# The first layer of a mixture of experts with weights standing and 128 tokens moving

## The chip, the cores and the metric

The program runs on one core of a Trainium2 chip. The metric is the device time in microseconds (us) of the whole program. Of its engines, TensorE (PE) multiplies, VectorE (DVE) and ScalarE (ACT) do arithmetic along partitions, GpSimd (POOL) starts gathers and scatters, and SyncE (SP) starts the plain transfers. In the profile PEld is the part of TensorE that loads the operand that stands.

## The reference: what is computed

Attention over 2 x 8 heads gives 1536 tokens of 512 numbers. A first mixture of 8 experts (two per token) follows, and then a second one, which is what the change touches. Its core is:

```python
def _moe2_ref(x, w_skip, w_gate, w1, w2):       # x 1536 x 512, w1 8 x 512 x 1024, w2 8 x 1024 x 512
    do_compute = x @ w_skip > 0                 # tokens that are computed at all
    out = x.copy(); xc = x[do_compute]
    logits = xc @ w_gate
    e_idx = np.argmax(logits, axis=1)           # one expert per token
    probs = softmax(logits); gate_w = probs[np.arange(len(xc)), e_idx]
    for e in range(8):
        mask = e_idx == e
        h = np.maximum(xc[mask] @ w1[e], 0.0)   # first layer: 1024 units
        y[mask] = gate_w[mask, None] * (h @ w2[e])
    out[do_compute] = xc + y
```

## The kernel before

Each engine has its own instruction list, written by hand in program order, and the lists meet at semaphores. No scheduler reorders anything. After the attention (to about 90 us of the profiled span), the routing of the first mixture (to 114 us), the first mixture (to 437 us) and the second routing (to 477 us), the second mixture runs to the end.

All products of the two mixtures are made from operands in the type F32R. A number is split in two: ACT rounds it to F32R (hi), DVE takes the rest (lo), and three products hi x hi, hi x lo and lo x hi are summed. Numbers of plain f32 are used only for turns (a product with the identity, which transposes 128 x 128) and for the small products of the routing.

The second mixture works in slots. A slot is up to 128 tokens of one expert; an expert with more tokens has more slots, and a register loop runs over them. In one slot, for the 128 tokens, PE does this (`second_mixture`, lines 951 to 1008):

1. First layer, `up`: for each of FH = 2 halves of 512 units, 12 products (4 chunks of the 512 inputs x 3 terms). The tokens stand (128 inputs x 128 tokens, `xt_hi`, `xt_lo`) and 512 columns of weights move. The result has tokens on partitions and 512 units along them, in one PSUM bank (`ps_h[half]`).
2. `turn_h`: the second layer sums over units, so these must lie on partitions. ACT applies the ReLU into `h_sb` (line 1282), PE turns four 128 x 128 pieces into `ps_ht[half]` (line 980), ACT rounds this into `ht_hi[half]` (line 1285) and DVE takes the rest into `ht_lo[half]` (line 1963). The turns of half 0 stand in the middle of the products of half 1, those of half 1 in the middle of the second layer's.
3. Second layer, `down`: 24 products, where `ht_hi` and `ht_lo` stand and 512 columns of the second weights move, into `ps_y`. Within it stands `turn_x` (line 936): the next slot's gathered rows `xg` are turned into `ps_xt`, which ACT rounds into `xt_hi` (line 1254) and of which DVE takes the rest into `xt_lo` (line 1935).

The helpers `terms` and `products` list the operands and issue the products; all of them have line 964. Before the first products of a slot PE waits only for half of `xt_hi`, after six for the other half, and for `xt_lo` before the last four of half 0. DVE then scales `ps_y` into `y_sb` (line 1973), and POOL scatters it. Beside this, ACT and DVE prepare the next expert's weights in 8 pieces (`round_next`, line 1097, and `split_next`, line 1615), placed between the steps of the slot by the table SLOT_PIECES = (2, 1, 2, 3).

Of the kernel before, what the change touches and what calls it, by code (L numbers as in the profile page):

```python
# [31 lines left out]
ALU = mybir.AluOpType  # L32
ACT = mybir.ActivationFunctionType
AX = mybir.AxisListType

P = 128
BATCH, HEADS, SEQ, HD = 2, 8, 768, 64
D = HEADS * HD
# [15 lines left out]
DK = D // P  # L54
FK = FF // P
FH = FF // D
# [95 lines left out]
def build(nc, q, k, v, gates1, gates2, noise, m1_w1, m1_w2, m2_w1, m2_w2, const, out):  # L152
# [14 lines left out]
    with keep:  # L167
# [3 lines left out]
        def sb_in(stack, name, shape, dt=F32):  # L171
            return stack.enter_context(nc.sbuf_tensor(name, shape, dt))
# [5 lines left out]
        bank = [keep.enter_context(nc.psum_tensor(f"bank{i}", [P, 512], F32))[:] for i in range(4)]  # L178
# [8 lines left out]

        TAIL = 2
        ps_gate_tail = bank[0]
        ps_h, ps_ht, ps_y, ps_xt = bank[0:2], bank[2:4], bank[4], bank[5]  # L190

        ps_unit, ps_out, ps_x, ps_turn = bank[0:2], bank[2:5] + [bank[6]], bank[5], bank[7]

# [10 lines left out]
        def c(name):  # L204
# [7 lines left out]
        ident = c("ident")  # L212
# [63 lines left out]
        routing = ExitStack()  # L276
# [32 lines left out]
        second = ExitStack()  # L309
        xt_b = [sb_in(second, f"xt_b{i}", [P, DK, P]) for i in range(2)]  # L310
        second.close()
        h_sb = sb_in(routing, "h_sb", [P, FH, D])
        ht_hi, ht_lo = [sb_in(routing, f"ht_{part}", [P, FH, DK, P], F32R) for part in ("hi", "lo")]
        xt_hi, xt_lo = [sb_in(routing, f"xt_{part}", [P, DK, P], F32R) for part in ("hi", "lo")]
        xg = sb_in(routing, "xg", [P, ROW])
# [92 lines left out]
            "gate": "DVE: the slot's gates are in gate_next (one more than slots)",  # L408
            "gated": "DVE: they are in gate_now",
            "h": "PE: one more half of the hidden layer",  # L410
            "relu": "ACT: in h_sb",
            "ht": "PE: transposed",
            "hth": "ACT: rounded, in ht_hi",
            "hte": "DVE: the rest is in ht_lo",
            "y": "PE: the expert's output (one more than slots)",
            "ix": "DVE: the slot's destinations are in ix_put",
            "set": "ACT: one more set of weights is free",
# [241 lines left out]
        def _(eng):  # L659
# [261 lines left out]
            def second_mixture():  # L921
                m, S = 1, slot_sems
                eng.sem_inc(S["xtp"], 1)
                eng.sem_inc(S["y"], 1)
                slot = eng.alloc_register(f"pe_slot{m}")
                eng.reg_mov(slot, 0)
                counts = [eng.alloc_register(f"pe_blocks{m}_{e}") for e in range(E)]
                done = eng.alloc_register(f"pe_done{m}")

                def turn_x(ahead, n):  # L930

                    eng.wait_ge(S["take"], (n + (ahead + 1)) * 16)
                    if ahead:
                        eng.wait_ge(S["xte"], n + ahead)
                    for i in range(DK):
                        last = eng.transpose(ps_xt[:, i * P:(i + 1) * P], xg[:, i * P:(i + 1) * P],  # L936
                                             ident)
                    last.then_inc(S["xtp"], 1)

                eng.wait_ge(s_counted, m + 1)  # L940
                eng.reg_load(counts, todo_i[0:1, 0:E])
                keep_warm(10, ps_y)
                turn_x(0, 0)

                eng.wait_ge(s_route, m + 1)
                for e in range(E):
                    n = m * E + e
                    hi, lo = w_hi[n % SETS], w_lo[n % SETS]
                    eng.wait_ge(s_lo, PIECES * n - PIECES // 2)
                    eng.reg_mov(done, 0)  # L950
                    with eng.While(lambda: eng.snap(done) < eng.snap(counts[e])):
                        sv = eng.snap(slot, min_val=0, max_val=2 * NT + E)

                        def terms(x_hi, x_lo, chunks):


                            with_hi = [(x_hi[i], w[:, chunk, :]) for i, chunk in enumerate(chunks)
                                       for w in (hi, lo)]
                            return with_hi + [(x_lo[i], hi[:, chunk, :])
                                              for i, chunk in enumerate(chunks)]  # L960

                        def products(ps, every, a, b):
                            for i in range(a, b):
                                last = eng.matmul(ps[:], *every[i], start=(i == 0),  # L964
                                                  stop=(i == len(every) - 1))
                            return last

                        xs = [[x[:, i, :] for i in range(DK)] for x in (xt_hi, xt_lo)]
                        up = [terms(*xs, [FH * i + half for i in range(DK)]) for half in range(FH)]
                        down = []  # L970
                        for half in range(FH):
                            hs = [[h[:, half, i, :] for i in range(DK)] for h in (ht_hi, ht_lo)]
                            down += terms(*hs, [WC // 2 + half * DK + i for i in range(DK)])
                        T = 3 * DK
                        H = 2 * DK

                        def turn_h(half):
                            eng.wait_ge(S["relu"], sv * 2 + (half + 1))
                            for i in range(DK):
                                last = eng.transpose(ps_ht[half][:, i * P:(i + 1) * P],  # L980
                                                     h_sb[:, half, i * P:(i + 1) * P], ident)
                            last.then_inc(S["ht"], 1)

                        eng.wait_ge(S["xth"], sv * 2 + 1)
                        products(ps_h[0], up[0], 0, H // 2)
                        eng.wait_ge(S["xth"], sv * 2 + 2)
                        products(ps_h[0], up[0], H // 2, H)
                        eng.wait_ge(S["xte"], sv + 1)
                        products(ps_h[0], up[0], H, T).then_inc(S["h"], 1)
                        products(ps_h[1], up[1], 0, T // 2)  # L990
                        turn_h(0)
                        products(ps_h[1], up[1], T // 2, T).then_inc(S["h"], 1)
                        eng.wait_ge(S["hth"], sv * 2 + 1)
                        eng.wait_ge(s_lo, PIECES * n)
                        eng.wait_ge(S["ye"], sv + 1)
                        products(ps_y, down, 0, T // 2)
                        turn_h(1)
                        products(ps_y, down, T // 2, H)
                        eng.wait_ge(S["hte"], sv * 2 + 1)
                        products(ps_y, down, H, T)  # L1000
                        eng.wait_ge(S["hth"], sv * 2 + 2)
                        products(ps_y, down, T, T + T // 3)
                        turn_x(1, sv)
                        products(ps_y, down, T + T // 3, T + H)
                        eng.wait_ge(S["hte"], sv * 2 + 2)
                        products(ps_y, down, T + H, 2 * T).then_inc(S["y"], 1)
                        eng.reg_add(slot, slot, 1)
                        eng.reg_add(done, done, 1)
# [68 lines left out]
        def _(eng):  # L1077
# [166 lines left out]
            def second_mixture():  # L1244
                m, S = 1, slot_sems
# [23 lines left out]
                for e in range(E):  # L1269
# [7 lines left out]
                    with eng.While(lambda: eng.snap(done) < eng.snap(counts[e])):  # L1277
                        sv = eng.snap(slot, min_val=0, max_val=2 * NT + E)
                        round_next(n, 0)
                        for half in range(FH):  # L1280
                            eng.wait_ge(S["h"], sv * 2 + (half + 1))
                            eng.activation(h_sb[:, half, :], ps_h[half][:], ACT.Relu)\
                               .then_inc(S["relu"], 1)
                            eng.wait_ge(S["ht"], sv * 2 + (half + 1))
                            eng.copy(ht_hi[:, half].rearrange("p k n -> p (k n)"), ps_ht[half][:])\
                               .then_inc(S["hth"], 1)
                            round_next(n, half + 1)
                        round_x(1, sv)
                        round_next(n, 3)
                        eng.reg_add(slot, slot, 1)  # L1290
                        eng.reg_add(done, done, 1)
# [278 lines left out]
        def _(eng):  # L1570
# [351 lines left out]
            def second_mixture():  # L1922
                m, S = 1, slot_sems
                eng.sem_inc(S["ye"], 1)
                slot = eng.alloc_register(f"dve_slot{m}")
                eng.reg_mov(slot, 0)
                counts = [eng.alloc_register(f"dve_blocks{m}_{e}") for e in range(E)]
# [22 lines left out]
                for e in range(E):  # L1950
# [3 lines left out]
                    with eng.While(lambda: eng.snap(done) < eng.snap(counts[e])):  # L1954
# [5 lines left out]
                        split_next(n, 0)  # L1960
                        for half in range(FH):
                            eng.wait_ge(S["hth"], sv * 2 + (half + 1))
                            eng.tensor_tensor(
                                ht_lo[:, half].rearrange("p k n -> p (k n)"), ps_ht[half][:],
                                ht_hi[:, half].bitcast(F32).rearrange("p k n -> p (k n)"),
                                ALU.subtract).then_inc(S["hte"], 1)
                            split_next(n, half + 1)
                        rest_of_x(1, sv)
                        split_next(n, 3)
# [84 lines left out]
```

## Time and profile before

| | us |
|---|---|
| time, median of 3 runs (lowest, highest) | 666.77 (666.35, 667.37) |
| time of the profiled execution | 665.87 |
| its span, from the first to the last instruction | 663.4 |
| PE busy in it | 620.8 (94%) |
| PEld busy | 551.5 (83%) |
| DVE busy | 367.9 (55%) |
| ACT busy | 293.9 (44%) |
| POOL busy | 237.9 (36%) |
| mean granted TensorE clock | 0.97 of full |

The span is cut in no stages by the profile; a stage is found by the lines that are active in it. A row of the timeline has its start, its length, the engine, the line, the operation, and the operands as out<-in; for a product the first operand after the arrow moves and the second stands, and "128x512" is the shape that moves. Products overlap in the pipe, so what one costs is the distance between the starts of two neighbours and not the length shown.

### The profile page before, as it was taken

To read this page: it belongs to the slowest core of one execution; us is meant where nothing else is said; L and a number is where in the kernel's file an instruction comes from. 1 tells how busy PE (TensorE), PEld (TensorE's weight loads), DVE (VectorE), ACT (ScalarE), POOL (GpSimd) and SP (SyncE) were. 2 spreads that over 40 slices of the span, in tenths; PEclk is the share of its full clock that TensorE was granted. 3 is DMA by queue.
4 is the path that set the end of the run, shared out by engine and by line. 5 is a ranking of instruction groups with operands and counts; after the bars stand their busy time and mean duration, and the time that the engine had idled before them with its cause. 6 is when DMAs were issued, how large, how long until landed. Compare 5 with 4: busy or idle time off the path is not lost.

```text
span 663.4 us, 13555 instructions
## 1 busy us (share of the span) xinstructions
PE 620.8 (94%) x4054; PEld 551.5 (83%) x4054; DVE 367.9 (55%) x714; ACT 293.9 (44%) x536; POOL 237.9 (36%) x223
## 2 busy tenths in 40 slices
PE   6888848999999999999999999998699999999994
PEld 6567735999999999999999999985478888888883
DVE  5759985644535554364644536423564687656641
ACT  2657732433424443253433434433255475646621
POOL 2558303105527063370725527033112223231230
PEclk9999967999999999999999999998699999999998
DMA  9999881442926448283672926885296679568220
GB/s 305 326 285 305 301 295 53 155 152 55 269 66 180 140 93 264 54 213 94 150 207 54 273 65 157 236 251 113 72 330 208 208 220 357 160 187 266 40 50 13
DMA packets 57633, 119.79 MB, mean 181 GB/s; under 512 B 13588, under 2 KB 13972, under 8 KB 57568
## 3 DMA queue, kind: packets, MB, share of 16 engines
q1 hardware_dynamic: 39424, 94.59, 43.4%
q0 software_dynamic: 14304, 23.93, 17.2%
q10 hardware_dynamic: 3840, 0.49, 0.5%
q8 instruction: 30, 0.49, 0.3%
q14 instruction: 35, 0.29, 0.1%
HBM read 103.51 MB, written 23.50 MB: 191 GB/s over the span
## 4 chain that ended last, share of the span: by engine, by line
PE 84%; DMA 5%; DVE 4%; issue 2%; SPq 2%; POOLq 0%; ACT 0%; POOL 0%; DVEq 0%; ACTq 0%
PE bank L964 22%; PE bank L856 22%; PE bank L850 22%; PE bank L839 2%; DMA q_ring<-in_q 2%; PE bank L819 2%; PE bank L745 2%; PE bank L980 2%; PE bank L724 1%; DMA xg<-x_moe,ix_take 1%; PE bank L768 1%; PE bank L758 1%; PE bank L713 1%; PE bank L936 1%; DVE col_val L1778 1%
## 5 line engine op out<-in xcount | busy, mean ns | idle before, releaser
L1615 DVE TENSOR_TENSOR w_lo<-stage,w_hi x120 | 141.7, 1222 | 22.9 <-ACT w_hi L1097 22.1
L1097 ACT CAST w_hi<-stage x120 | 119.7, 1050 | 9.0 <-PE bank L964 8.9
L856 PE MATMUL bank<-unit_hi,w_hi 128*128 128x416 f32 x256 | 92.6, 362 | 0.0
L1873 DVE SCALAR_TENSOR_TENSOR unit_lo<-bank,unit_hi 128x416 fp32r<-128x416 f32 x64 | 37.9, 592 | 96.8 <-ACT unit_hi L1211 96.8
L850 PE MATMUL bank<-tok_hi,w_hi 128*128 128x416 f32 x256 | 90.5, 354 | 0.6 <-DVE tok_lo L1825 0.6
L1211 ACT ACTIVATE unit_hi<-bank 128x416 fp32r<-128x416 f32 x64 | 33.2, 519 | 129.9 <-PE bank L850 129.9
L856 PE MATMUL bank<-unit_lo,w_hi 128*128 128x416 f32 x256 | 90.2, 352 | 0.0
L850 PE MATMUL bank<-tok_hi,w_lo 128*128 128x416 f32 x256 | 89.7, 350 | 0.0
L856 PE MATMUL bank<-unit_hi,w_lo 128*128 128x416 f32 x256 | 89.7, 350 | 0.0
L1429 POOL DMA_INDIRECT x_more<-more_out,ix_put x32 | 51.6, 1614 | 42.2 <-DVE more_out L1844 26.3
L1441 POOL DMA_INDIRECT x_moe<-rows_out,ix_put x32 | 55.2, 1726 | 9.8 <-issue 9.8
L850 PE MATMUL bank<-tok_lo,w_hi 128*128 128x416 f32 x256 | 58.5, 350 | 0.0
L1409 POOL COPY ix_take<-take_ix 128x4 int32 (+1 forms) x8 | 1.5, 184 | 135.2 <-PE bank L819 135.2
L850 PEld LDWEIGHTS bank<-tok_hi,w_hi 128*128 128x128 f32 x256 | 48.0, 188 | 1.5 <-issue 1.0
L856 PEld LDWEIGHTS bank<-unit_hi,w_hi 128*128 128x128 f32 x256 | 48.1, 188 | 1.0
L856 PEld LDWEIGHTS bank<-unit_hi,w_lo 128*128 128x128 f32 x256 | 48.3, 189 | 0.5
L850 PEld LDWEIGHTS bank<-tok_hi,w_lo 128*128 128x128 f32 x256 | 48.1, 188 | 0.4
L856 PEld LDWEIGHTS bank<-unit_lo,w_hi 128*128 128x128 f32 x256 | 48.0, 188 | 0.4
L850 PEld LDWEIGHTS bank<-tok_lo,w_hi 128*128 128x128 f32 x256 | 47.9, 187 | 0.5
L964 PE MATMUL bank<-w_hi,ht_hi 128*128 128x512 f32 x112 | 46.7, 417 | 0.0
L964 PE MATMUL bank<-w_hi,xt_hi 128*128 128x512 f32 x112 | 45.6, 407 | 0.5 <-ACT xt_hi L1254 0.5
L964 PE MATMUL bank<-w_lo,ht_hi 128*128 128x512 f32 x112 | 44.3, 395 | 0.0
(162 smaller groups left out, 1072.5 us busy)
## 6 DMA issues: line engine op xcount, KB each, us to landing
stage<-in_moe_w SPq DMA_DIRECT2D x128, 512.0 KB, 5.6
v_win<-in_v SPq DMA_DIRECT2D x24, 198.0 KB, 8.9
v_raw<-in_v SPq DMA_DIRECT2D x6, 528.0 KB, 13.4
x_moe<-rows_out SPq DMA_DIRECT2D x12, 260.0 KB, 3.6
kt<-in_k SPq DMA_DIRECT2D x8, 384.0 KB, 9.0
q_ring<-in_q SPq DMA_DIRECT2D x6, 512.0 KB, 9.6
x_att<-x_sb POOLq DMA_DIRECT2D x12, 256.0 KB, 5.8
x_part<-x_moe SPq DMA_DIRECT2D x4, 768.0 KB, 8.8
```

The source lines that it names most:

```text
L745: last = eng.matmul(ps_heads[part, h, 0:HD + 1], pt_sb[:, s % 2, i, part], v_win[:, (2 * t + half) % WR, h * VD:(h + 1) * VD], start=True, ...
L819: last = eng.transpose(ps[:, i * rows:(i + 1) * rows], rows_in[0:rows, t, i * P:(i + 1) * P], ident[0:rows, 0:rows])
L839: last = eng.transpose(ps_turn[0:PART[t], t * P:(t + 1) * P], out_t[:, PSTART[t]:PSTART[t] + PART[t]], ident)
L850: last = eng.matmul(ps_unit[f % 2][:, 0:W], w, x, start=(i == 0), stop=(i == len(mine) - 1))
L856: last = eng.matmul(ps_out[chunk][:, 0:W], w[:, WC // 2 + f, chunk * P:(chunk + 1) * P], h[:, f % UNITS, :], start=(f == 0 and i == 0), st ...
L964: last = eng.matmul(ps[:], *every[i], start=(i == 0), stop=(i == len(every) - 1))
L1097: eng.copy(piece(w_hi[n % SETS], j), stage[:, j, :]).then_inc(s_hi, 1)
L1211: eng.activation(unit_hi[:, f % UNITS, :], ps_unit[f % 2][:, 0:W], ACT.Relu)\
L1429: eng.indirect_dma_start(more_dram, bass.IndirectOffsetOnAxis(ap=ix_put[0:rows, t:t + 1], axis=0), more_out[0:rows, t, :], None, bounds_ch ...
L1441: eng.indirect_dma_start(x1_dram, bass.IndirectOffsetOnAxis(ap=ix_put[0:rows, t:t + 1], axis=0), rows_out[0:rows, t, :], None, bounds_chec ...
L1615: eng.tensor_tensor(piece(w_lo[n % SETS], j), stage[:, j, :], piece(w_hi[n % SETS], j).bitcast(F32), ALU.subtract)\
L1873: eng.scalar_tensor_tensor(unit_lo[:, f % UNITS, :], ps_unit[f % 2][:, 0:W], 0.0, unit_hi[:, f % UNITS, :].bitcast(F32), ALU.max, ALU.subt ...
```

## The change

In the first layer the operands trade places. For each half and each of its four groups of 128 units, 12 products are made in which a 128 x 128 piece of the weights stands and the 128 tokens move, into 128 columns of `ps_h[half]`. The result has units on partitions, so that `turn_h`, `h_sb`, `ps_ht` and the semaphores "relu" and "ht" go. ACT applies the ReLU and rounds to F32R in one instruction from `ps_h`, and DVE takes max(x, 0) - hi from the same bank. PE now waits for all of `xt_hi` and `xt_lo` before its first product, and for DVE to have read `ps_h[half]` of the slot before; ACT waits for the last slot's output before it writes `ht_hi`.

```diff
@@ PE, second_mixture
-                        xs = [[x[:, i, :] for i in range(DK)] for x in (xt_hi, xt_lo)]
-                        up = [terms(*xs, [FH * i + half for i in range(DK)]) for half in range(FH)]
+                        def units(half):
+                            for at in range(0, D, P):
+                                every = [(w[:, FH * i + half, at:at + P], x[:, i, :])
+                                         for x, ws in ((xt_hi, (hi, lo)), (xt_lo, (hi,)))
+                                         for i in range(DK) for w in ws]
+                                for i, (w, x) in enumerate(every):
+                                    last = eng.matmul(ps_h[half][:, at:at + P], w, x, start=(i == 0),
+                                                      stop=(i == len(every) - 1))
+                            last.then_inc(S["h"], 1)
...
-                        eng.wait_ge(S["xth"], sv * 2 + 1)
-                        products(ps_h[0], up[0], 0, H // 2)
                         eng.wait_ge(S["xth"], sv * 2 + 2)
-                        products(ps_h[0], up[0], H // 2, H)
                         eng.wait_ge(S["xte"], sv + 1)
-                        products(ps_h[0], up[0], H, T).then_inc(S["h"], 1)
-                        products(ps_h[1], up[1], 0, T // 2)
-                        turn_h(0)
-                        products(ps_h[1], up[1], T // 2, T).then_inc(S["h"], 1)
+                        eng.wait_ge(S["hte"], sv * 2 + 1)
+                        units(0)
+                        eng.wait_ge(S["hte"], sv * 2 + 2)
+                        units(1)
                         eng.wait_ge(S["hth"], sv * 2 + 1)
                         eng.wait_ge(s_lo, PIECES * n)
                         eng.wait_ge(S["ye"], sv + 1)
-                        products(ps_y, down, 0, T // 2)
-                        turn_h(1)
-                        products(ps_y, down, T // 2, H)
-                        eng.wait_ge(S["hte"], sv * 2 + 1)
+                        products(ps_y, down, 0, H)
+                        eng.wait_ge(S["hte"], sv * 2 + 3)
                         products(ps_y, down, H, T)
@@ ACT, second_mixture
                             eng.wait_ge(S["h"], sv * 2 + (half + 1))
-                            eng.activation(h_sb[:, half, :], ps_h[half][:], ACT.Relu)\
-                               .then_inc(S["relu"], 1)
-                            eng.wait_ge(S["ht"], sv * 2 + (half + 1))
-                            eng.copy(ht_hi[:, half].rearrange("p k n -> p (k n)"), ps_ht[half][:])\
-                               .then_inc(S["hth"], 1)
+                            eng.wait_ge(S["y"], sv + 1)
+                            eng.activation(ht_hi[:, half].rearrange("p k n -> p (k n)"), ps_h[half][:],
+                                           ACT.Relu).then_inc(S["hth"], 1)
@@ DVE, second_mixture
-                            eng.tensor_tensor(
-                                ht_lo[:, half].rearrange("p k n -> p (k n)"), ps_ht[half][:],
+                            eng.scalar_tensor_tensor(
+                                ht_lo[:, half].rearrange("p k n -> p (k n)"), ps_h[half][:], 0.0,
                                 ht_hi[:, half].bitcast(F32).rearrange("p k n -> p (k n)"),
-                                ALU.subtract).then_inc(S["hte"], 1)
+                                ALU.max, ALU.subtract).then_inc(S["hte"], 1)
```

On PE, in the second half of the first layer and the start of the second, this stood in a row before (w_hi and w_lo are the weights' two parts, xt the tokens, ht the turned hidden layer, h_sb the layer not yet turned):

```order
L964 MATMUL bank<-w_hi,xt_hi 128x512
L964 MATMUL bank<-w_lo,xt_hi 128x512
L964 MATMUL bank<-w_hi,xt_hi 128x512
L964 MATMUL bank<-w_lo,xt_hi 128x512
L964 MATMUL bank<-w_hi,xt_hi 128x512
L964 MATMUL bank<-w_lo,xt_hi 128x512
L980 MATMUL bank<-c_late,h_sb 128x128 x4
L964 MATMUL bank<-w_hi,xt_hi 128x512
L964 MATMUL bank<-w_lo,xt_hi 128x512
L964 MATMUL bank<-w_hi,xt_lo 128x512 x4
L964 MATMUL bank<-w_hi,ht_hi 128x512
```

And this stands on PE now for the last 128 units of the second half and the start of the second layer:

```order
L966 MATMUL bank<-xt_hi,w_hi 128x128
L966 MATMUL bank<-xt_hi,w_lo 128x128
L966 MATMUL bank<-xt_hi,w_hi 128x128
L966 MATMUL bank<-xt_hi,w_lo 128x128
L966 MATMUL bank<-xt_hi,w_hi 128x128
L966 MATMUL bank<-xt_hi,w_lo 128x128
L966 MATMUL bank<-xt_hi,w_hi 128x128
L966 MATMUL bank<-xt_hi,w_lo 128x128
L966 MATMUL bank<-xt_lo,w_hi 128x128 x4
L972 MATMUL bank<-w_hi,ht_hi 128x512
L972 MATMUL bank<-w_lo,ht_hi 128x512
```

Twelve products of 512 moving columns for 512 units became four such groups of twelve, with 128 moving columns each, and the operand that stands changes from tokens to weights; the turns are gone.

On ACT, from a slot's first to its last step of its own, this stood before (the pieces of the next weights, which stand between, are left out of this last expert's slot):

```order
L1282 ACTIVATE h_sb<-bank 128x512
L1285 CAST ht_hi<-bank 128x512
L1281 REGISTER_ALU
L1282 ACTIVATE h_sb<-bank 128x512
L1285 CAST ht_hi<-bank 128x512
L1252 REGISTER_ALU
L1254 CAST xt_hi<-bank 128x256 x2
```

and this now:

```order
L1276 REGISTER_ALU
L1277 ACTIVATE ht_hi<-bank 128x512
L1275 REGISTER_ALU
L1277 ACTIVATE ht_hi<-bank 128x512
L1246 REGISTER_ALU
L1248 CAST xt_hi<-bank 128x256 x2
```

Two of ACT's four passes over the hidden layer are gone, and the one left in each half writes `ht_hi` itself.

## Rows read from the trace of the kernel before

**Rows 1.** The page: the chain that ended last, shares of the span by line.

```profile
PE bank L964 22%; PE bank L856 22%; PE bank L850 22%; PE bank L839 2%; DMA q_ring<-in_q 2%; PE bank L819 2%; PE bank L745 2%; PE bank L980 2%; PE bank L724 1%; DMA xg<-x_moe,ix_take 1%; PE bank L768 1%; PE bank L758 1%; PE bank L713 1%; PE bank L936 1%; DVE col_val L1778 1%
```

**Rows 2.** Busy by stretch: length, PE, PEld, DVE, ACT, POOL, clock, DMA, GB/s.

```profile
489.80:652.80 163.00, 163.00 (x782) 132.44 (x781) 100.30 (x143) 87.44 (x129) 44.20 (x39) 1.00 0.61 192
33.00:83.00 50.00, 43.80 (x707) 36.96 (x705) 41.56 (x71) 33.72 (x93) 29.97 (x41) 1.00 0.95 298
472.60:474.50 1.90, 1.84 (x4) 1.49 (x5) 0.66 (x3) 0.00 (x0) 1.10 (x1) 0.50 0.00 0
```

**Rows 3.** Chain of waits, one slot: start us, us, what.

```profile
502.33 6.07 PE bank L964 x26
508.84 2.81 PE bank L964 x12
514.85 6.08 PE bank L964 x26
```

**Rows 4.** Groups by form on PE: count, busy us, mean ns.

```profile
L964 PE MATMUL bank<-w_hi,xt_hi 128*128 128x512 f32 x112 | 45.6, 407 | 0.5 <-ACT xt_hi L1254 0.5
L980 PE MATMUL bank<-c_late,h_sb 128*128 128x128 f32 x112 | 16.8, 273 | 0.0
```

**Rows 5.** Timeline, slot 2: start us, us, engine, line, operation.

```profile
491.54 0.39 PE L964 MATMUL bank<-w_hi,xt_hi 128*128 128x512 f32 x1
...
493.17 0.39 PE L964 MATMUL bank<-w_lo,xt_hi 128*128 128x512 f32 x1
...
496.06 0.19 PEld L964 LDWEIGHTS bank<-w_hi,xt_hi 128*128 128x128 f32 x1
496.17 0.19 PEld L964 LDWEIGHTS bank<-w_lo,xt_hi 128*128 128x128 f32 x1
496.41 0.40 PE L964 MATMUL bank<-w_lo,xt_hi 128*128 128x512 f32 x1
```

**Rows 6.** Timeline of the first mixture, 416 columns a product.

```profile
124.16 0.19 PEld L856 LDWEIGHTS bank<-unit_hi,w_lo 128*128 128x128 f32 x1
124.35 0.35 PE L856 MATMUL bank<-unit_hi,w_lo 128*128 128x416 f32 x1
```

**Rows 7.** Timeline: plain f32 products, 16 columns moving.

```profile
38.10 0.97 PEld L758 LDWEIGHTS bank<-wgate,xt_a 128*128 128x128 f32 x8
```

**Rows 8.** Timeline: plain f32 products, 128 columns moving.

```profile
441.29 1.04 PE L768 MATMUL bank<-xt_b,wgate 128*9 128x128 f32 x8 [0.24 <-ACT xt_b L1174]
```

**Rows 9.** Weight loads by line: ns min/median/max, first and last start.

```profile
L693 PEld LDWEIGHTS bank<-w_hi x30: 186/330/338, 104.8 to 476.2; 128*128 128x128 f32 x30
...
L758 PEld LDWEIGHTS bank<-wgate,xt_a x96: 186/192/338, 33.2 to 88.1; 128*128 128x128 f32 x96
```

**Rows 10.** Timeline: tokens of slot 3, from their turn to their use.

```profile
502.37 0.65 ACT L1254 CAST xt_hi<-bank 128x256 fp32r<-128x256 f32 x2 [2.17 <-PE bank L936]
503.13 0.68 DVE L1935 TENSOR_TENSOR xt_lo<-bank,xt_hi 128x512 fp32r<-128x512 f32 x1
504.05 0.40 PE L964 MATMUL bank<-w_hi,xt_hi 128*128 128x512 f32 x1
```

**Rows 11.** Timeline: the first slot's start, and the wait within it.

```profile
478.11 0.50 PE L964 MATMUL bank<-w_hi,xt_hi 128*128 128x512 f32 x1 [0.46 <-ACT xt_hi L1254]
478.45 0.68 DVE L1935 TENSOR_TENSOR xt_lo<-bank,xt_hi 128x512 fp32r<-128x512 f32 x1
...
489.16 0.66 PE L936 MATMUL bank<-c_late,xg 128*128 128x128 f32 x4 [0.56 <-DMA xg<-x_moe,ix_take]
```

**Rows 12.** ACT and DVE by form, within one slot.

```profile
L1963 DVE TENSOR_TENSOR ht_lo<-bank,ht_hi 128x512 fp32r<-128x512 f32 x2 | 1.4, 692 | 1.5 <-ACT ht_hi L1285 1.5
...
L1282 ACT ACTIVATE h_sb<-bank 128x512 f32<-128x512 f32 x2 | 1.2, 604 | 0.3 <-PE bank L964 0.3
L1285 ACT CAST ht_hi<-bank 128x512 fp32r<-128x512 f32 x2 | 1.2, 588 | 2.4 <-PE bank L980 2.4
```

**Rows 13.** The page: the same DVE form, from the first mixture.

```profile
L1873 DVE SCALAR_TENSOR_TENSOR unit_lo<-bank,unit_hi 128x416 fp32r<-128x416 f32 x64 | 37.9, 592 | 96.8 <-ACT unit_hi L1211 96.8
```

More of the change, by code:

```diff
@@ L189, in build @@
         ps_gate_tail = bank[0]
-        ps_h, ps_ht, ps_y, ps_xt = bank[0:2], bank[2:4], bank[4], bank[5]
+        ps_h, ps_y, ps_xt = bank[0:2], bank[4], bank[5]
         ps_unit, ps_out, ps_x, ps_turn = bank[0:2], bank[2:5] + [bank[6]], bank[5], bank[7]
@@ L311, in build @@
         second.close()
-        h_sb = sb_in(routing, "h_sb", [P, FH, D])
         ht_hi, ht_lo = [sb_in(routing, f"ht_{part}", [P, FH, DK, P], F32R) for part in ("hi", "lo")]
@@ L410, in build @@
             "h": "PE: one more half of the hidden layer",
-            "relu": "ACT: in h_sb",
-            "ht": "PE: transposed",
             "hth": "ACT: rounded, in ht_hi",
-            "hte": "DVE: the rest is in ht_lo",
+            "hte": "DVE: the rest is in ht_lo (two more)",
             "y": "PE: the expert's output (one more than slots)",
@@ L952, in second_mixture, with terms @@
                         sv = eng.snap(slot, min_val=0, max_val=2 * NT + E)
-                        def terms(x_hi, x_lo, chunks):
-                            with_hi = [(x_hi[i], w[:, chunk, :]) for i, chunk in enumerate(chunks)
+                        def terms(h_hi, h_lo, chunks):
+                            with_hi = [(h_hi[i], w[:, chunk, :]) for i, chunk in enumerate(chunks)
                                        for w in (hi, lo)]
-                            return with_hi + [(x_lo[i], hi[:, chunk, :])
+                            return with_hi + [(h_lo[i], hi[:, chunk, :])
                                               for i, chunk in enumerate(chunks)]
+                        def units(half):
[7 more added lines that the diff above has]
+                            last.then_inc(S["h"], 1)
                         def products(ps, every, a, b):
@@ L975, in second_mixture @@
                         H = 2 * DK
[L977 to L982, printed above, removed]
-                        eng.wait_ge(S["xth"], sv * 2 + 1)
-                        products(ps_h[0], up[0], 0, H // 2)
                         eng.wait_ge(S["xth"], sv * 2 + 2)
-                        products(ps_h[0], up[0], H // 2, H)
                         eng.wait_ge(S["xte"], sv + 1)
-                        products(ps_h[0], up[0], H, T).then_inc(S["h"], 1)
-                        products(ps_h[1], up[1], 0, T // 2)
-                        turn_h(0)
-                        products(ps_h[1], up[1], T // 2, T).then_inc(S["h"], 1)
+                        eng.wait_ge(S["hte"], sv * 2 + 1)
+                        units(0)
+                        eng.wait_ge(S["hte"], sv * 2 + 2)
+                        units(1)
                         eng.wait_ge(S["hth"], sv * 2 + 1)
@@ L1004, in second_mixture @@
                         products(ps_y, down, T + T // 3, T + H)
-                        eng.wait_ge(S["hte"], sv * 2 + 2)
+                        eng.wait_ge(S["hte"], sv * 2 + 4)
                         products(ps_y, down, T + H, 2 * T).then_inc(S["y"], 1)
@@ L1924, in second_mixture @@
                 eng.sem_inc(S["ye"], 1)
+                eng.sem_inc(S["hte"], 2)
                 slot = eng.alloc_register(f"dve_slot{m}")
```

## The prediction, made before the result was known

> **What bounds the kernel now.** I read the shares of the chain of waits first. It names PE lines at its head, and the line of the second mixture's products (964) has 22% of the span [rows 1]. Then the busy time by stretch: in the 163.00 us that hold 13 slots PE is busy 163.00, at a granted clock of 1.00 (the higher of its two levels, 2.4 GHz), while DVE has 100 and ACT 87 [rows 2]. So a slot is as long as PE's own instructions, and any time put on PE or taken off it in a slot moves the end by the same. The chain of one slot shows this: from 502.33 to 514.85 it is PE with no gap of another engine worth a row, 12.52 us [rows 3]. The number of slots: the product of w_hi with xt_hi occurs 8 times a slot (2 halves x 4 chunks) and 112 times in all [rows 4], so there are 14 slots.
>
> **What a 512-column product and a turn cost.** The lengths shown overlap, so I take distances. From 491.54 to 493.17 there are seven steps: 1.63 / 7 = 0.233 us [rows 5]. A slot has 48 such products, 11.18 us. The other 12.52 - 11.18 = 1.34 us are 12 turns, 0.112 us each.
>
> **What goes from PE.** 24 products of the first layer, 24 x 0.233 = 5.59 us, and the eight turns of `turn_h` (8 x 14 = 112, as counted [rows 4]), 8 x 0.112 = 0.90 us. Together 6.49 us a slot.
>
> **What comes to PE.** 2 halves x 4 groups x 12 = 96 products with 128 columns moving and 128 x 128 F32R standing. The arithmetic is the same as that of the 24; if only columns counted, a product would cost 0.233 / 4 = 0.058 us. But each one needs another piece to stand, so 96 loads stand where 24 stood, and before, the 512 columns that moved hid each load. The trace has no F32R product with fewer than 416 columns, so its price must be bounded.
> - From below: 0.058 us, by columns alone.
> - By the load: after the turns, where PE has two loads to make at once, two F32R loads start at 496.06 and 496.17, so one load holds the next up for 0.11 us [rows 5]. Plain f32 pieces of the same 128 x 128, with only 16 columns moving, show it better: eight loads take 0.97 us [rows 7], the last one alone 0.19 (median 192 ns [rows 9]), so their starts are (0.97 - 0.19) / 7 = 0.111 us apart.
> - From above: plain f32 with 128 columns moving has two records a product, and eight records take 1.04 us [rows 8], so a product costs 0.22 (starts apart, with the last one's 0.27 us taken off, the length of a 128-column product [rows 4]) to 0.26 us.
>
> I take 0.111, the nearest row: same piece standing, same bytes, few columns moving. 96 x 0.111 = 10.66 us.
>
> On this the Trainium skill's page "TensorE: Matmul & The Clock Gate" (section "Back-to-back issue gap") speaks more kindly: in a sustained stream of loads and products it gives about 81 ns for each product of 128 columns. By it the 96 would cost 7.8 us, an estimate, and not 10.66. The trace has only spacings of 0.11 for 128 columns of 4-byte numbers, so I keep it as a rival.
>
> **The sum.** A slot gains 10.66 - 6.49 = 4.17 us on PE, 14 slots 58.4 us.
>
> **Edits off PE.** ACT loses two passes a slot (588 ns each) and keeps two (604); DVE's pass keeps its cost: the subtraction takes 692 ns for 512 columns [rows 12], the form that is new here took 592 for 416 in the first mixture [rows 13]. ACT and DVE have room, 87 and 100 us of 163 [rows 2], and a longer slot gives more. This is hidden work: 0.
>
> **New waits.** PE's first product now waits for all of `xt_lo`, and everything of PE is queued behind it. In slot 3 the rounding starts 502.37, the rest 503.13 and lasts 0.68, to 503.81; the first product of the slot starts 504.05 [rows 10]. The stretch behind `turn_x` on PE (8 products) stays, so the 0.24 us of slack stays. In slots where DVE's pieces of weights delayed the rest, they stood behind a half that itself waited for a turn; that turn is gone, so they come sooner. I take 0, and at most 0.3 us a slot, 4 us in all. Below nothing it cannot go, since a wait gives nothing back. In the first slot the start moves: product at 478.11, `xt_lo` ready at 478.45 + 0.68 = 479.13 [rows 11], so 1.0 us more. Its wait of 0.56 us for gathered rows at 489.16 [rows 11] goes, because PE now comes there some 4 us later. Net 0.5. The wait for `ps_h` is for a read that ended in the slot before; ACT's new wait for "y" is met when the products that it reads begin. Both 0.
>
> Total 58.4 + 0.5 = 58.9 us. The profiled execution took 665.87 us, so 724.8; the median of the runs is 0.9 higher, so about **725.7 us**.
>
> **Rivals.**
> - *Columns price it, not slower.* If loads hid fully, 0.058 x 96 = 5.6 us against 6.49, so 0.9 less a slot, 12.9 us in all: 654 us. It takes the place of the load's cost in the first layer, and decides below 6.49 / 96 = 0.0676 us a product. For it: nowhere in the mixture did a load cost anything. Against: both spacings of 0.11. Chance 0.03.
> - *Loads partly hidden.* A product costs between 0.0676 and 0.10 us, because F32R loads pipeline better than the plain ones; with 0.081 it is 7.78 - 6.49 = 1.29 a slot, 18 us: 685 us. Against it stands the 0.11 of the two F32R loads themselves. Chance 0.06. It would take the page's figure to be right for 4-byte pieces.
> - *Loads in series.* In the first mixture a load starts at 124.16, lasts 0.19, and its product starts at 124.35 [rows 6]; if a load may not start before the product before it, and must end before its own, the spacing is 0.19. Then 96 x 0.19 = 18.2, 11.7 more a slot, 164 in all: 831 us. Against it: 496.06 and 496.17, two loads that overlap, and the eight of [rows 7]. Chance 0.08.
> - *F32R is fast only with many columns moving.* All 128-column products of 4-byte numbers here cost like plain ones, and all F32R products shown move 416 or 512. If 128 columns fall back to the price of plain f32, 0.22 us a product, a slot gains 21.1 - 6.49 = 14.6 us, 205 in all: 872 us. For it: nothing here excludes it. Against: no row shows such a fall. Chance 0.24. The Trainium skill's page "FP8 and Floating Point Precision" (section "TensorE Precision Notes") gives plain f32 four passes and has reduced f32 read 4 bytes and cut them to 22 bits, with no word on columns; by it the 872 would not come, and the sum would stay with the load. No run so far shows which.
> - *The clock falls.* The moving side is now at work about half the time of the first layer (0.058 of 0.111). With the clock at 0.50 [rows 2] an F32R load has 330 ns instead of 186 [rows 9]; twice the spacing, 0.222 us, again gives 872 us. Against: in the attention, with short products all along and PE busy 43.8 of 50 us, the clock was 1.00 [rows 2]. Chance 0.03.
>
> **How the numbers follow.** The forecast has 0.56. Its own range: 0.108 to 0.120 us a product (0.120 being the F32R surplus that 0.233 has over 512 columns at 2.4 GHz, 9%, laid on the load) and 0 to 4 us of waits, so 720 to 742 us. The two slow prices hold 0.35 with the clock's, so a range that leaves out 2 in 10 must reach them: 716 to 885 us, 0.91 of the chance, the lower rivals left out. Faster by over 0.2% (about what a measurement of this kernel can tell from no change) only in the first rival, part of it: 0.02. Within 0.2%: 0.01. Slower: 0.97, which all others share.
>
> **What would show it.** Right: in the first layer starts 0.11 us apart, load behind load, PE busy all through, slots of 16.7 us, the granted clock at 1.00, the second layer's products still 0.233 apart, no waits on ACT or DVE at a slot's start but for the first. Wrong: a first layer of about 5.6 us (columns), 18 (series) or 21 (plain price); lengths of records that grow from 0.27 us tell the plain price from the load, since a longer pass shows in the product and a longer load in PEld. The step on which all hangs is the 0.111.

## The result, and the profile after

The changed kernel takes 735.51 us (median of 4 runs, 734.39 to 738.41), the kernel before 667.07 us on the same chip (4 runs, 666.35 to 668.41). The ratio is 1.106, with a 95% interval of 1.103 to 1.110. The forecast was 726 us with a range of 716 to 885. All ratios in this document are of executions within 1.5% of the fastest one of their kernel.

The page of the changed kernel: the shares of the chain by line, and the groups of the new first layer on PE, PEld, DVE and ACT (out<-in, count, busy us, mean ns, idle before).

```profile
PE bank L966 22%; PE bank L853 20%; PE bank L847 20%; PE bank L972 11%; PE bank L836 2%; PE bank L742 2%; PE bank L816 2%; PE bank L721 2%; PE bank L710 1%; DMA v_raw<-in_v 1%; PE bank L755 1%; PE bank L765 1%; PE bank L672 1%; PE bank L933 1%; DVE col_val L1770 1%
...
L966 PE MATMUL bank<-xt_hi,w_hi 128*128 128x128 f32 x448 | 110.3, 283 | 1.6 <-DVE xt_lo L1928 1.6
L966 PEld LDWEIGHTS bank<-xt_hi,w_hi 128*128 128x128 f32 x448 | 89.9, 201 | 4.1 <-issue 4.1
...
L1956 DVE SCALAR_TENSOR_TENSOR ht_lo<-bank,ht_hi 128x512 fp32r<-128x512 f32 x28 | 19.4, 691 | 89.3 <-ACT ht_hi L1277 89.3
...
L1277 ACT ACTIVATE ht_hi<-bank 128x512 fp32r<-128x512 f32 x28 | 16.8, 598 | 118.0 <-PE bank L966 118.0
```

The products of the first layer (now line 966, 22% of the span) and of the second (972, 11%) stand in the chain in place of the common line 964, which had 22% [rows 1]. DVE's new form takes 691 ns against 692 before, and ACT's one pass 598 ns [rows 12]. Both engines wait more than before, and behind the first slot's start they hold up PE nowhere (the 1.6 us that PE waits for `xt_lo` in line 966 are all at that start): the edits off PE cost nothing, as forecast.

The chain of waits from the first slot into the third (start us, us, what):

```profile
477.07 0.69 DVE xt_lo L1928
477.88 19.87 PE bank L966 x96
497.75 6.10 PE bank L972 x16
506.17 10.67 PE bank L966 x96
516.84 3.78 PE bank L972 x16
521.06 1.86 PE bank L972 x8
522.92 10.68 PE bank L966 x96
```

From 506.17 to 522.92 one slot takes 16.75 us: 10.67 for 96 products (0.111 each), 5.64 for 24 of 512 columns (3.78 and 1.86), the rest the four turns of the tokens. It took 12.52 us before [rows 3]. All the later slots look alike, 16.77 us on average. The first slot does not: from 477.88 to 506.17 it takes 28.29 us.

PEld in a later slot, four loads of the first layer in a row (start us, us):

```profile
539.43 0.19 PEld L966 LDWEIGHTS bank<-xt_hi,w_hi 128*128 128x128 f32 x1 [0.16 <-issue]
539.55 0.19 PEld L966 LDWEIGHTS bank<-xt_hi,w_lo 128*128 128x128 f32 x1
539.66 0.19 PEld L966 LDWEIGHTS bank<-xt_hi,w_hi 128*128 128x128 f32 x1
539.77 0.19 PEld L966 LDWEIGHTS bank<-xt_hi,w_lo 128*128 128x128 f32 x1
```

The starts are 0.11 us apart while each load is shown with 0.19: loads overlap, and a new one starts every 0.11 us. That the product waits for its load, and not for something else that costs 0.11 us, is what the table by columns below is for. Before, the same two starts, 0.11 apart, stood only where PE came out of its turns [rows 5].

The granted clock on PE in the first slot (window, length, PE busy and count, PEclk, DMA share, GB/s):

```profile
core 0: us, PE busy (x), PEclk, DMA share, GB/s
475.00:476.00 1.00, 1.00 (x6) 0.78 0.01 4
477.00:478.00 1.00, 0.12 (x1) 1.00 0.83 262
478.00:479.00 1.00, 1.00 (x10) 0.93 1.06 393
479.00:480.00 1.00, 1.00 (x6) 0.50 1.08 342
480.00:484.00 4.00, 4.00 (x21) 0.50 1.00 301
504.00:508.00 4.00, 4.00 (x30) 1.00 0.33 115
```

The clock rises to 1.00 (2.4 GHz) between 475 and 476, in the last of the ten wide products that warm PE up ahead of the slots. PE idles for 1.6 us, until 477.88. Its clock is still 1.00 then, falls to 0.50 (1.2 GHz) at about 479, and stays there through all of the narrow products; it is back by 504, after products of 512 columns have run from 497.6. The 96 products take 19.87 us there and not 10.67, and the second layer's first 16 take 6.10 and not 3.78. In all later slots the clock is at 1.00 (columns: length, PE, PEld, DVE, ACT, POOL, PEclk, DMA share, GB/s):

```profile
506.17:722.00 215.83, 215.83 (x1604) 200.41 (x1603) 100.05 (x140) 70.79 (x100) 42.15 (x38) 1.00 0.45 133
```

So the 69.5 us between the two profiled executions (735.36 - 665.87) are: 13 later slots, 13 x (16.77 - 12.54) = 55.0, where 12.54 is the 163.00 us of [rows 2] over 13; the first slot, 28.13 against 13.43, 14.7; an earlier start, 477.88 against 478.11, -0.2. Both lengths of the first slot are from its first product to that of the second slot: to 506.01 now, where the chain's piece begins 0.16 later, and from 478.11 to 491.54 before, with the wait for gathered rows in it [rows 5, 11].

### The profile page after: what moved, and what is told of

It is laid out like the page before. It is cut to its first block, busy times and chain, and to the rows that moved or that the text cites. A ratio compares the mean times of both kernels' runs of the same rounds, so it can differ in the third digit from the quotient of the medians.

```text
span 732.9 us, 15376 instructions
## 1 busy us (share of the span) xinstructions
PE 690.1 (94%) x4950; PEld 637.4 (87%) x4950; DVE 371.6 (51%) x714; ACT 278.1 (38%) x508; POOL 236.2 (32%) x223
## 4 chain that ended last, share of the span: by engine, by line
PE 89%; DVE 4%; DMA 3%; issue 2%; SPq 1%; ACT 0%; POOLq 0%; POOL 0%; DVEq 0%; ACTq 0%
PE bank L966 22%; PE bank L853 20%; PE bank L847 20%; PE bank L972 11%; PE bank L836 2%; PE bank L742 2%; PE bank L816 2%; PE bank L721 2%; PE bank L710 1%; DMA v_raw<-in_v 1%; PE bank L755 1%; PE bank L765 1%; PE bank L672 1%; PE bank L933 1%; DVE col_val L1770 1%
## 5 line engine op out<-in xcount | busy, mean ns | idle before, releaser
L966 PE MATMUL bank<-xt_hi,w_hi 128*128 128x128 f32 x448 | 110.3, 283 | 1.6 <-DVE xt_lo L1928 1.6
L966 PE MATMUL bank<-xt_hi,w_lo 128*128 128x128 f32 x448 | 110.8, 283 | 0.0
L966 PEld LDWEIGHTS bank<-xt_hi,w_hi 128*128 128x128 f32 x448 | 89.9, 201 | 4.1 <-issue 4.1
L966 PEld LDWEIGHTS bank<-xt_hi,w_lo 128*128 128x128 f32 x448 | 89.9, 201 | 0.0
L966 PE MATMUL bank<-xt_lo,w_hi 128*128 128x128 f32 x448 | 71.9, 285 | 0.0
L1956 DVE SCALAR_TENSOR_TENSOR ht_lo<-bank,ht_hi 128x512 fp32r<-128x512 f32 x28 | 19.4, 691 | 89.3 <-ACT ht_hi L1277 89.3
L966 PEld LDWEIGHTS bank<-xt_lo,w_hi 128*128 128x128 f32 x448 | 62.5, 202 | 0.0
L1277 ACT ACTIVATE ht_hi<-bank 128x512 fp32r<-128x512 f32 x28 | 16.8, 598 | 118.0 <-PE bank L966 118.0
L1497 POOL COPY ix_take<-take_ix 128x1 int32 (+1 forms) x14 | 2.6, 185 | 156.4 <-DVE gate_next L1927 156.4
```

The costliest lines, as they stand in the source:

```text
L966: last = eng.matmul(ps_h[half][:, at:at + P], w, x, start=(i == 0), stop=(i == len(every) - 1))
L1277: eng.activation(ht_hi[:, half].rearrange("p k n -> p (k n)"), ps_h[half][:], ACT.Relu).then_inc(S["hth"], 1)
L1956: eng.scalar_tensor_tensor(ht_lo[:, half].rearrange("p k n -> p (k n)"), ps_h[half][:], 0.0, ht_hi[:, half].bitcast(F32).rearrange("p k n ...
```

## The experiments

Two questions were open: what a narrow product's price is made of, and what took the clock in the first slot. Times of kernels in different sets of runs are compared through the kernel before, which ran beside each set (667.07, 666.54 and 665.27 us).

### Wide products in the gap

```diff
                 keep_warm(10, ps_y)
                 turn_x(0, 0)
+                keep_warm(7, ps_y)
```

> The changed kernel with seven more F32R products of 512 columns on PE behind the first turn of tokens, where PE now sits idle for 1.6 us until the rest of the tokens is ready. Idle theory (that gap, which the new wait made, let the granted clock fall to 0.50, and the narrow stream of the first layer keeps a clock but does not win it back): the clock stays 1.00, the first slot takes 16.8 us and not 28.3, and the time is 735.5 - 11.5 = 724 us. Stream theory (the narrow products of the first slot lose the clock by themselves): the clock falls again within the first slot, 735 us. Neither touches the later slots, 16.77 us each.

Measured: 724.14 us (722.52 to 724.38), ratio to before 1.087 (1.084 to 1.091), where the changed kernel has 1.106 (1.103 to 1.110). Clock by window on PE, and the chain of the first slot:

```profile
477.00:478.00 1.00, 1.00 (x12) 1.00 1.10 346
480.00:484.00 4.00, 4.00 (x38) 1.00 0.99 276
```

```profile
476.18 10.91 PE bank L967 x96
487.09 3.79 PE bank L973 x16
491.31 1.88 PE bank L973 x8
493.19 10.67 PE bank L967 x96
```

The clock stays at 1.00, and the first slot, 476.18 to 493.19, takes 17.0 us. Without the gap the narrow stream keeps the clock, as the idle theory had it, and the stream theory falls. Some 11 us of the change's cost were the clock of one slot.

### Narrow work in the gap

```diff
                 turn_x(0, 0)
+                keep_busy(15, ps_y)
```

> The changed kernel with fifteen plain turns of the identity (128 columns) in the same gap in place of wide products, about 1.6 us of them at 0.11. Idle theory: anything that fills the gap will do, 724 us. Stream theory: narrow work loses the clock, in the gap or behind it, 735 us. If only the wide filling helps, what runs in the gap matters and not that something runs.

Measured: 724.96 us (722.03 to 729.31), ratio 1.090 (1.085 to 1.096). The clock on PE:

```profile
474.00:475.00 1.00, 1.00 (x12) 1.00 0.29 31
480.00:484.00 4.00, 4.00 (x38) 1.00 0.97 239
```

In the profiled execution fifteen turns of the identity do as well as seven wide products: what counted was that PE was at work, wide or narrow. Two of the four executions took 727 and 729 us, some 5 more than the other two; they have no trace, so what they lost is open.

### One half of the first layer alone

```diff
-                        products(ps_h[0], up[0], ...)     # tokens stand, 512 columns
+                        units(0)                          # weights stand, 128 columns
                         products(ps_h[1], up[1], 0, T).then_inc(S["h"], 1)
...
+                                eng.activation(ht_hi[:, 0] ..., ps_h[0][:], ACT.Relu)   # half 0, ACT
```

> One part of the change alone: half 0 of the first layer has the weights standing, half 1 is as before (tokens stand, turned by PE, the turns in the second layer). Load theory: a slot has 48 narrow products x 0.111 = 5.33 us in place of 12 x 0.233 + 4 x 0.112 = 3.24 us, 2.09 more, 29 us in 14 slots: 696 us, and if the first slot falls to the low clock as well, until the wide products have run, some 5 to 10 more, 701 to 706. If the cost were in the new waits or at a slot's start and not in the count of products, it would be nearly that of the whole change, 725 to 735.

Measured: 703.51 us (700.7 to 705.17), ratio 1.055 (1.050 to 1.059). Its chain:

```profile
478.67 10.36 PE bank L983 x48
...
515.15 5.31 PE bank L983 x48
...
530.05 5.57 PE bank L983 x48
```

A later slot takes 530.05 - 515.15 = 14.90 us, 2.4 more than before, where 2.1 were expected; the narrow products are at 5.31 / 48 = 0.111 again. A piece of 5.57 us begins with a product that had to wait: in 7 of these slots PE sits idle for about 0.25 us until `xt_lo` is there, 1.7 us in all, about half of what the 13 later slots have above the sum (0.3 us each). So the cost goes with the number of narrow products and not with the fact of the change.

The first slot is at the low clock here too: 48 narrow products take 10.36 us. PE had waited for 1.6 us ahead of the first one, at 478.67. The clock on PE:

```profile
478.00:479.00 1.00, 0.33 (x2) 0.93 0.93 295
479.00:480.00 1.00, 1.00 (x7) 0.50 1.03 393
```

With 0.93 on average between 478 and 479 it fell in the last 0.15 us or so of that stretch, when no more than two narrow products had started. So here the narrow stream can hardly have been what took the clock; the narrow products only ran at the low one and did not bring it back.

### The price by columns

```diff
             second_mixture()
+            for cols in (512, 448, 416, 384, 320, 288, 256, 224, 192, 160, 128, 96, 64):
+                for i in range(4):      # 512 columns, to have the same start for each block
+                    eng.matmul(ps_turn[:], w_hi[1][:, 0, 0:P], w_hi[1][:, 1, :], start=True, stop=True)
+                for i in range(24):
+                    eng.matmul(ps_turn[:, 0:cols], w_hi[1][:, i % 8, 0:P], w_hi[1][:, 1, 0:cols],
+                               start=True, stop=True)
```

> The kernel before, with blocks of F32R products on PE behind its last slot (extra work, no part of the result): 24 products each, every one with another 128 x 128 piece standing, and 512, 448, 416, 384, 320, 288, 256, 224, 192, 160, 128, 96 and 64 columns moving, four of 512 columns ahead of each block. Load theory: the distance between starts is the larger of 0.111 us and 0.000455 us a column, so it falls to about 245 columns and is flat at 0.111 below. Plain-price theory (F32R costs as plain f32 below some number of columns): a jump up, to 0.22 at 128 columns, which the changed kernel already speaks against. Series theory: flat at 0.19 below 416.

There is one execution, of 712.6 us, and only distances within it are read. The loads on PEld of the blocks with 512, 416, 256, 224, 128 and 64 columns, in this order (start us, us in all, count):

```profile
653.90 5.40 PEld L1079 LDWEIGHTS bank<-w_hi 128*128 128x128 f32 x24
...
666.03 4.57 PEld L1079 LDWEIGHTS bank<-w_hi 128*128 128x128 f32 x24
...
685.10 3.04 PEld L1079 LDWEIGHTS bank<-w_hi 128*128 128x128 f32 x24
...
688.89 2.88 PEld L1079 LDWEIGHTS bank<-w_hi 128*128 128x128 f32 x24
...
699.67 2.87 PEld L1079 LDWEIGHTS bank<-w_hi 128*128 128x128 f32 x24
...
706.89 2.88 PEld L1079 LDWEIGHTS bank<-w_hi 128*128 128x128 f32 x24
```

Less the last load's own 0.19 us and over 23 steps, the loads start 0.227 us apart with 512 columns, 0.190 with 416, 0.124 with 256, and 0.117 with 224, 128 or 64. But the first load of a block stands behind a wide product, and the step from it to the second is 0.23 us in every block (699.67 to 699.90 in the one with 128 columns). From the second load on, the blocks with 256 and 128 columns read:

```profile
685.33 2.81 PEld L1079 LDWEIGHTS bank<-w_hi 128*128 128x128 f32 x23
...
699.90 2.64 PEld L1079 LDWEIGHTS bank<-w_hi 128*128 128x128 f32 x23
```

Over 22 steps that is 0.119 us with 256 columns and 0.111 with 128, and in the same way 0.189 with 416, 0.112 with 224 and 0.111 with 64. The cost falls with the columns to somewhere between 256 and 224 and is flat below, at the 0.111 of the slots. The granted clock was 1.00 from 652 to 709 us. There is no jump up at few columns and no floor at 0.19: the plain-price and the series rivals fall.

A flat floor could also be a fixed price of any product, whatever stands. The trace of the kernel before has the counterexample, in the second routing: six products with 128 columns moving and a 128 x 128 piece standing, each with a load of its own, but in f16, two bytes a number (granted clock 1.00).

```profile
464.56 0.51 PE L804 MATMUL bank<-col_val,lane_hot 128*128 128x128 f16 x6
```

Less the last one's 0.22 us, their starts are 0.058 us apart, what 128 columns alone would cost by [rows 5]. Nor is it the four-byte numbers that move: in the block of 512, 128 of them cost 0.227 / 4 = 0.057 us. So the 0.111 us are those of a standing 128 x 128 piece of four-byte numbers.

### The wait alone, in the kernel before

```diff
-                        eng.wait_ge(S["xth"], sv * 2 + 1)
-                        products(ps_h[0], up[0], 0, H // 2)
                         eng.wait_ge(S["xth"], sv * 2 + 2)
-                        products(ps_h[0], up[0], H // 2, H)
                         eng.wait_ge(S["xte"], sv + 1)
-                        products(ps_h[0], up[0], H, T).then_inc(S["h"], 1)
+                        products(ps_h[0], up[0], 0, T).then_inc(S["h"], 1)
```

> The kernel before with one part of the change alone: PE waits for all of the tokens, rounded and rest, before the first product of a slot. The first layer and its turns are as before. If that wait is the cause of the low clock by the idle time that it makes, the clock falls to 0.50 here too, and the question is how long the wide products take to win it back: some 5 us at the low clock cost 2.5 us, with 1.1 us for the later start and up to 4 us where a slot's tokens are late, 668 to 674 us. If the low clock needs the narrow products as well, only the wait itself is paid: 667 to 670 us.

Measured: 667.64 us against 665.27, ratio 1.0035 (1.0015 to 1.0055). The clock on PE through the gap and behind it, and what the first products waited for in all slots:

```profile
478.00:479.20 1.20, 0.04 (x1) 1.00 0.94 340
479.20:482.00 2.80, 2.80 (x12) 1.00 1.05 347
```

```profile
L964 PE MATMUL bank<-w_hi,xt_hi 128*128 128x512 f32 x112 | 46.2, 413 | 3.0 <-DVE xt_lo L1932 3.0
```

PE is idle about as long as in the changed kernel (1.5 us ahead of the product at 479.16), and the clock does not fall: a gap of this length does not take it every time. The mean clock of all six executions (0.970 to 0.973) is that of the kernel before in the same set (0.965 to 0.974), while the four of the changed kernel are at 0.956 to 0.961. What made the difference is not shown. It may be the narrow work behind the gap, but in the run with one half the clock fell almost as that work began. It may be how long the clock had been up: here it rose between 477 and 478, just ahead of the gap, and in the changed kernel between 475 and 476, with wide products and turns behind it. What holds in both traces with a low clock is that a gap stood ahead of narrow products, and that these did not bring the clock back. The wait itself costs 3.0 us of idle time here, in 7 of the 14 slots. In the changed kernel, the page has one such wait, the 1.6 us of the first slot (the last column of line 966 above). That ACT and DVE come to the tokens in time there because they no longer wait for turns is argued, not tried.

### Half the columns, the same loads

```diff
                                 for i, (w, x) in enumerate(every):
-                                    last = eng.matmul(ps_h[half][:, at:at + P], w, x, ...)
+                                    cols = P if i == 0 else P // 2
+                                    last = eng.matmul(ps_h[half][:, at:at + cols], w, x[:, 0:cols], ...)
```

> The changed kernel with 64 moving columns in 11 of every 12 products of the first layer and 128 in the first (the other 64 tokens get only the first of their 12 terms). The loads are the same 96. Load theory: no change, 735 us, the products still start 0.111 us apart. Column theory (0.000455 us a column, with something constant added): 88 x 64 x 0.000455 = 2.6 us less a slot, 36 us in all, 699 us.

Measured: 835.13 us (three executions, 831.32 to 836.33; a fourth took 844.51), ratio 1.253 (1.250 to 1.257). Neither theory had that. The first layer of one slot in its chain, then the starts of products of 64 columns within it, two before and two after the clock fell, and the clock:

```profile
556.78 17.14 PE bank L967 x96
```

```profile
559.90 0.28 PE L967 MATMUL bank<-xt_hi,w_hi 128*128 128x64 f32 x1
560.01 0.28 PE L967 MATMUL bank<-xt_hi,w_lo 128*128 128x64 f32 x1
...
562.00 0.40 PE L967 MATMUL bank<-xt_hi,w_lo 128*128 128x64 f32 x1
562.21 0.40 PE L967 MATMUL bank<-xt_hi,w_hi 128*128 128x64 f32 x1
```

```profile
560.00:561.00 1.00, 1.00 (x8) 0.59 1.07 413
```

While the clock is at 1.00 the products start 0.11 us apart, as with 128 columns, which is what the load theory says. Shortly after 560 it falls to 0.50 with no gap at all, and the distance becomes 0.21. In each slot the second layer's wide products bring the clock back, and the narrow ones lose it again. Taking work away made the kernel some 100 us slower.

### A third of the loads taken away

```diff
-                                every = [(w[...], x[:, i, :]) for x, ws in ((xt_hi, (hi, lo)), (xt_lo, (hi,))) ...]
+                                for i in range(DK):
+                                    both = xt_both[:, i].rearrange("p a n -> p (a n)")   # xt_hi and xt_lo, 256 columns
+                                    eng.matmul(aside[:, ...2 * P], hi[w_here], both, ...)
+                                    eng.matmul(aside[:, ...P], lo[w_here], xt_hi[:, i, :], ...)
```

> The changed kernel with its gap filled by seven wide products (724.1 us), and a third of the loads of the first layer taken away: each piece of the weights' rounded part stands once and both parts of the tokens move past it, 256 columns, where they took two products of 128. 64 products in place of 96, the same columns. (The sum of the two results is not made, and ACT and DVE read only one bank of the two in which they now lie, as much as before.) Load theory, with the prices of the table: 32 x 0.124 + 32 x 0.111 = 7.5 us in place of 10.7, 3.1 less a slot, 44 in all: 680 us. Column theory: no change, 724 us. In neither does it come under the 667 us of the kernel before.

The gap is filled with seven wide products here too, so it compares with the 724.14 us of that run. Measured: 678.99 us (674.53 to 681.78), ratio 1.020 (1.016 to 1.023). The second layer of two slots in its chain:

```profile
503.16 3.78 PE bank L979 x16
507.37 1.88 PE bank L979 x8
516.56 3.78 PE bank L979 x16
```

A slot is 516.56 - 503.16 = 13.40 us, so its first layer takes 13.40 - 6.10 = 7.30 us for 64 products (the 6.10 being 16.77 - 10.67, what the second layer and the tokens' turns take). The same columns with 32 loads fewer save 3.4 us a slot, 45 us in all. The load theory had 3.1 and 44 with 0.124 us for 256 columns (3.3 a slot with 0.119), the column theory nothing. It also shows the limit of this layout: even so, the first layer costs more than the 6.49 us of the old one with its turns, and no version here comes under the kernel before.

## Why the prediction came out as it did

- **What bounds the kernel**: right. PE's time in a slot moved the end one for one.
- **What goes**: 6.49 us a slot, and **what comes**: 96 x 0.111 = 10.66. Measured 10.67, and a slot grew by 4.2 us where 4.17 were forecast. The step on which all hung, the 0.111 of a load from [rows 5, 7], held to the nanosecond that the views give. The table by columns, the pairs and the f16 products show that it is the load.
- **Edits off PE at 0**: right.
- **New waits**: right in size for the later slots (0) and in the first (0.5 forecast for the later start less the wait for gathered rows). The wait for the rows at 489 is gone. But the wait was priced only as time: "In the first slot the start moves [...] so 1.0 us more." It left PE idle for 1.6 us where it had been 0.46 [rows 11], and the slot behind that gap ran at the low clock: 28.13 us against 16.77, 11.4 us. This term was missing from the sum: 58.9 + 11.4 = 70.3 would have been the sum, against 69.5 between the profiled executions.
- **The range**: part luck. Its inner part, 720 to 742 us, holds the 735.5, but it was made for a product of up to 0.120 us and waits of up to 4 us. The products came out at 0.111 and the later waits at 0; what carried the time 10 us above the forecast was the clock of one slot, for which the inner part had no term.
- **The clock rival** (0.03) came near, but let the narrow work take the clock by itself, in all slots or none. At 128 columns it kept the clock in 13 slots and lost it in the one behind a gap; by itself it lost it only at 64. The evidence used against the rival, the attention at 1.00 [rows 2], was of narrow work that had the clock already; it said nothing of winning it back. It was also of one execution: in the trace of the changed kernel the attention runs at 0.50 from 80 to 82 us, on code that the change does not touch.
- **Loads partly hidden, or columns alone**: wrong, 0.111 stood. The 81 ns that the Trainium skill's page "TensorE: Matmul & The Clock Gate" gives (section "Back-to-back issue gap") do not hold for F32R pieces: 0.111 us a product wherever the clock was at 1.00.
- **Loads in series, and the plain price**: wrong by the 0.111 and by the table. The upper part of the range, up to 885, was there for them.

## What to carry to other kernels

A product costs about the larger of its moving columns and the load of the piece that stands, so which operand stands is decided by how many loads each order needs: here 96 against 24, for eight turns saved. For F32R here the two are equal between 224 and 256 columns; with 128 tokens and 512 columns of weights the tokens should stand. And a wait put ahead of narrow products must be priced with the clock, not with its length alone: keep PE at work through it, as seven wide products and fifteen turns both did here.

## What the runs showed of the hardware

- F32R, 128 x 128 standing: a product costs 0.111 us from 224 columns down to 64, in the table as in the slots, and from 256 up it follows the columns: 0.119 at 256, 0.189 at 416, 0.227 at 512. The same 128 columns with an f16 piece of 128 x 128 standing cost 0.058.
- The clock by what PE had done: products of 128 columns at 0.111 us kept it at 1.00 for 10.67 us in each of 13 slots; behind 1.6 us of idle time it fell, 1 us after they had begun in one kernel and about 0.2 us after in another, and they did not win it back in 19.87 us with PE busy throughout; a gap of 1.5 us ahead of products of 512 columns did not lower it. Products of 64 columns lost it in mid-stream with no gap. So a share of 100% busy on PE does not say that the clock holds. Where between 64 and 128 columns this turns, how long a gap it takes, and what sets the gaps that cost the clock apart from the one that did not, was not tried.
